# Attention and two MLPs: norm weight folded into a matrix, row-tiled transposes, one threshold on GpSimd, one addition on ScalarE

## What is computed

```python
scores = q @ k.T / 8
keep   = scores >= max(scores) - tau
attn   = where(keep, exp(scores - max), 0);  attn /= sum(attn) + 1e-9
x      = attn @ v                                     # 2304 x 512

h    = x @ w_in1                                      # 512 -> 1024
solu = h * softmax(h)
ln   = (solu - mean(solu)) / sqrt(var(solu) + 1e-6) * g_ln
y    = ln @ w_out1                                    # 1024 -> 512

m = y @ w_in2                                         # 512 -> 2048
g = max(m, 0) + log(1 + exp(-|m|))
out = g @ w_out2                                      # 2048 -> 512
```

## Time and profile before

| | us |
|---|---|
| median of 3 runs | 910.83 (910.66 to 911.72) |
| the profiled execution | 911.15 |
| its span, first to last instruction | 909.4 |
| TensorE busy | 869.7 (96%) |
| VectorE busy | 762.1 (84%) |
| ScalarE busy | 501.7 (55%) |
| GpSimd busy | 433.4 (48%) |
| mean granted TensorE clock, share of full speed | 0.994 |

### The profile page before, as it was taken

How to read it: one execution, slowest core, us unless ns; L and a number is a source line. 1 busy time by engine, 2 the same in 40 slices (tenths; PEclk the granted TensorE clock), 3 DMA queues, 4 the chain that set the end, 5 groups by cost and what they waited for, 6 DMA issues and landing times.

```text
span 909.4 us, 16546 instructions
## 1 busy us (share of the span) xinstructions
PE 869.7 (96%) x6104; PEld 726.3 (80%) x6104; DVE 762.1 (84%) x1376; ACT 501.7 (55%) x936; POOL 433.4 (48%) x449
## 2 busy tenths in 40 slices
PE   6899999999989999999998998999999999999997
PEld 4566666666667889889898897999989999899995
DVE  6999999999929754835641999999999999999997
ACT  4777877888846442433442564545545455455543
POOL 3445444447617612313311565565555556556563
PEclk9999999999999999999999899999999999999999
DMA  6813431342100000000002610000000000000000
GB/s 163 217 32 80 102 97 37 80 105 75 48 25 23 24 1 1 1 1 1 1 12 88 197 30 0 36 1 1 35 1 1 35 1 1 35 0 0 35 0 35
DMA packets 29496, 37.65 MB, mean 41 GB/s; under 512 B 3696, under 2 KB 17520, under 8 KB 29424
## 3 DMA queue, kind: packets, MB, share of 16 engines
q1 hardware_dynamic: 29024, 36.42, 14.5%
q10 hardware_dynamic: 400, 0.30, 0.1%
HBM read 31.98 MB, written 4.72 MB: 40 GB/s over the span
## 4 chain that ended last, share of the span: by engine, by line
DVE 53%; PE 35%; issue 8%; POOL 1%; ACT 1%; DMA 0%; ACTq 0%; DVEq 0%; POOLq 0%
DVE g L850 12%; PE y_ps L1044 11%; DVE ntop L710 8%; PE s_ps L942 7%; DVE g_hi L854 7%; DVE g L840 5%; PE h_ps L911 5%; DVE g_lo L856 5%; DVE g L843 5%; PE o_ps L982 4%; PE f_ps L1101 3%; PE m_ps L1020 2%; DVE x_lo L705 2%; DVE solu L807 1%; DVE st_top L793 1%
## 5 line engine op out<-in xcount | busy, mean ns | idle before, releaser
L451 POOL TENSOR_TENSOR w_lo<-w_raw,w_hi 128x512 fp32r<-128x512 f32 x96 | 129.6, 1351 | 163.6 <-ACT w_hi L632 163.6
L412 POOL TENSOR_SCALAR kept<-kept,inv 128x576 f32<-128x576 f32 x144 | 106.1, 756 | 117.9 <-DVE inv L742 117.8
L511 ACT ACTIVATE expd<-s_ps,ntop 128x576 f32<-128x576 f32 x144 | 106.3, 741 | 51.7 <-DVE ntop L710 51.7
L1020 PE MATMUL m_ps<-y_hi,w_lo 128*128 128x384 f32 x384 | 131.4, 342 | 0.0
L648 ACT ACTIVATE l<-u 128x384 f32<-128x384 f32 x96 | 50.4, 525 | 145.8 <-POOL u L459 145.8
L1020 PE MATMUL m_ps<-y_lo,w_hi 128*128 128x384 f32 x384 | 130.3, 339 | 0.0
L1020 PE MATMUL m_ps<-y_hi,w_hi 128*128 128x384 f32 x384 | 129.2, 336 | 0.0
L459 POOL TENSOR_TENSOR u<-z,consts 128x384 f32<-128x384 f32 x96 | 108.2, 1127 | 41.8 <-ACT z L641 41.7
L850 DVE TENSOR_TENSOR g<-g,l 128x384 f32<-128x384 f32 x96 | 125.7, 1309 | 2.7
L1101 PE MATMUL f_ps<-w_hi,g_hi 128*128 128x512 f32 x288 | 115.4, 401 | 8.9 <-DVE g_lo L856 8.9
L710 DVE TENSOR_REDUCE ntop<-s_ps 128x1 f32<-128x576 f32 x144 | 107.5, 757 | 14.2 <-PE s_ps L942 6.8
(11 more groups left out here) (87 smaller groups left out, 1815.1 us busy)
## 6 DMA issues: line engine op xcount, KB each, us to landing
q_sb<-q_t SPq DMA_DIRECT2D x28, 288.0 KB, 5.1
v_sb<-v_main SPq DMA_DIRECT2D x16, 256.0 KB, 3.2
stage<-w_in SPq DMA_DIRECT2D x16, 256.0 KB, 2.7
w_raw<-w_out SPq DMA_DIRECT2D x8, 512.0 KB, 4.8
out<-o_sb SPq DMA_DIRECT2D x5, 768.0 KB, 3.5
k_sb<-k_t SPq DMA_DIRECT2D x21, 144.0 KB, 4.4
stage<-w_in SPq DMA_DIRECT2D x4, 512.0 KB, 8.9
stage<-w_out SPq DMA_DIRECT2D x4, 512.0 KB, 3.7
```

The costliest lines, as they stand in the source:

```text
L412: nc.gpsimd.tensor_scalar(kept[:, tile % RING, :], kept[:, tile % RING, :], inv[:, group % 2, k:k + 1], 1.0, ALU.mult, ALU.mult).then_inc( ...
L451: nc.gpsimd.tensor_tensor(w4[1][:, n % 2, :], w4_raw[:, n % F2, :], f32(w4[0][:, n % 2, :]), ALU.subtract).then_inc(w4lo_made, 1)
L511: nc.scalar.activation(expd[:, tile % 2, :].rearrange("p (a b) -> p a b", a=2), s_ps[tile % 2][:, :, 0:HALF], ACT.Exp, bias=ntop[:, tile % ...
L1020: last = nc.tensor.matmul(m_ps[n % 4][:, 0:GC], w[:, k, (n % F2) * P:(n % F2 + 1) * P], y[odd][:, k, :], start=(k == 0 and m == 0), stop=( ...
```

## The change

Four edits are made together.

- The weight g_ln is multiplied into the rows of w_out1 (`w2_scale`, on ScalarE, in place in the stage buffers, in the last doubles of attention) before that matrix is split. VectorE's z is gone; GpSimd makes ln = (solu + nmean) * rstd in one operation. `solu` now waits for `ln_made`, and ln for `lt_made`. The gain is loaded as 128x8 near the start instead of as 128x1024 after attention.
- The transposes of the first MLP are 16 instructions on 64-row tiles, one tile's outputs in one bank of `lt_ps` and the other's in the other; `ln_hi` and `ln_lo` are addressed to match.
- In attention the second threshold of a double is made by GpSimd, with a semaphore of its own (`thresh_b`), and the reduction of the sums of even groups stands at the end of the double. The key scalings and w1's halves move on GpSimd and ScalarE.
- 1 + z of the second MLP is a ScalarE activation (Identity with bias 1) instead of a GpSimd addition.

```diff
-            for group in range(GROUPS):
+            def make_threshold_b(u):
+                pool.wait_ge(top_made, 2 * u + 2)
+                col = slice((2 * u + 1) % 4, (2 * u + 1) % 4 + 1)
+                nc.gpsimd.tensor_scalar(thresh[:, col], ntop[:, col], -1.0, tau_sb[:, 0:1], ALU.mult, ALU.subtract
+                                        ).then_inc(thresh_b, 1)
+            for u in range(DOUBLES + 1):
+                if u < DOUBLES:
+                    make_threshold_b(u)
+                for group in complete(u - 1):
+                    probabilities(group)
+                unit, step = divmod(u, PT)
+                if step == PT - 2 and unit + 1 < UNITS:
+                    scale_keys(2 * unit + 2)
+                    scale_keys(2 * unit + 3)
+                if u in W1_LOW:
+                    for m in range(2):
+                        w1_low(2 * W1_LOW.index(u) + m)
...
-                pool.wait_ge(z_made, tile + 1)
-                nc.gpsimd.tensor_tensor(ln[:, slot, :], ln[:, slot, :],
-                                        st["rstd"][:, col].broadcast_to([P, DFF1]), ALU.mult).then_inc(ln_made, 1)
+                pool.wait_ge(mean_made, tile + 1)
+                wait(pool, lt_made, tile - 1)
+                nc.gpsimd.tensor_scalar(ln[:, slot, :], solu[:, slot, :], st["nmean"][:, col], st["rstd"][:, col],
+                                        ALU.add, ALU.mult).then_inc(ln_made, 1)
...
+            def w2_scale(n):
+                src, hi, lo = staged(n)
+                act.wait_ge(stage_in[n % STAGES], 16 * (n // STAGES + 1))
+                act.wait_ge(gain_in, 16)
+                for a in range(2):
+                    m = 2 * (n - C) + a
+                    nc.scalar.activation(src[:, a, :], src[:, a, :], ACT.Copy, scale=gain[:, m:m + 1]
+                                         ).then_inc(w2_scaled, 1)
...
-                if 54 <= v < 54 + 2 * C:
-                    w1_high(v - 54)
+                if 24 <= v < 24 + 3 * C and v % 3 < 2:
+                    w1_high(2 * (v // 3 - 8) + v % 3)
+                if DOUBLES <= v < DOUBLES + F1 // 2:
+                    w2_scale(C + v - DOUBLES)
...
+            def one_plus(j, n):
+                slot = n % 2
+                act.wait_ge(z2_made, j + 1)
+                wait(act, l2_made, j - 1)
+                nc.scalar.activation(u2[:, slot, :], z2[:, slot, :], ACT.Identity, bias=consts[:, 3:4]
+                                     ).then_inc(u2_made, 1)
...
-                dve.wait_ge(thresh_made, tile + 1)
+                dve.wait_ge((thresh_a, thresh_b)[tile % 2], tile // 2 + 1)
...
+                    wait(dve, ln_made, tile - 1)
                     nc.vector.scalar_tensor_tensor(out=solu[:, slot, :], in0=h_ps[slot][:, :],
...
-                    nc.vector.scalar_tensor_tensor(out=ln[:, slot, :], in0=solu[:, slot, :],
-                                                   scalar=st["nmean"][:, col], in1=gain[:, :],
-                                                   op0=ALU.add, op1=ALU.mult).then_inc(z_made, 1)
...
                 for k in range(F1):
-                    last = nc.tensor.transpose(lt_bank(tile)[:, k * P:(k + 1) * P], ln[:, slot, k * P:(k + 1) * P],
-                                               ident[:, :])
+                    for q in range(2):
+                        last = nc.tensor.matmul(lt_bank(tile)[:, q * BANK + k * DH:q * BANK + (k + 1) * DH],
+                                                ln[halves[q], slot, k * P:(k + 1) * P],
+                                                ident[halves[q], q * DH:(q + 1) * DH], is_transpose=True,
+                                                start=(k == 0), stop=(k == F1 - 1))
```

More of the change, by code:

```diff
@@ L48 @@
 LAG_V = 6
+W1_LOW = (28, 31, 37, 40)
 BANK = 512
@@ L102, in build @@
         consts = sb("consts", [P, 5])
+        gain = sb("gain", [P, F1])
         xt = sb("xt", [P, 2 * PG * C * GC])
@@ L142, in build @@
         ln = sb("ln", [P, 2, DFF1], where=phase)
-        gain = sb("gain", [P, DFF1], where=phase)
         e1 = sb("e1", [P, 2, DFF1], where=phase)
@@ L241, in x_group, with complete @@
             return (b * PG + g) * (C * GC)
+        def complete(u):
+            return [group for group in range(GROUPS) if (GROUP * group + GROUP - 1) // 2 == u]
         def place(tile):
@@ L266, in lt_bank, with lt_halves, in_halves @@
             return h_ps[1] if isinstance(tile, int) and tile == MT - 2 else lt_ps
+        def lt_halves(tile):
+            return lt_bank(tile)[:, :].rearrange("p (q a b) -> p q a b", q=2, a=F1)
+        def in_halves(rows, k):
+            return rows[:, :, k * P:(k + 1) * P].rearrange("p a (q b) -> p q a b", q=2)
         W_ITEMS = C + F1 // 2 + F2
@@ L337, in _ @@
                 sp.dma_start(staged(n)[0], staged_source(n)).then_inc(stage_in[n], 16)
+            sp.dma_start(gain[:, :], gain_d.rearrange("(k p) -> p k", p=P),
+                         allow_slow_non_contiguous=True).then_inc(gain_in, 16)
             for unit in range(2, UNITS):
@@ L405, in _, with probabilities @@
                                             ALU.mult, ALU.mult).then_inc(k_scaled, 1)
-            for group in range(GROUPS):
+            def make_threshold_b(u):
[3 more added lines that the diff above has]
+                                        ).then_inc(thresh_b, 1)
+            def probabilities(group):
@@ L409, in _ @@
                 pool.wait_ge(inv_made, group + 1)
-                for k in range(GROUP):
-                    tile = GROUP * group + k
+                for tile in range(GROUP * group, GROUP * group + GROUP):
                     nc.gpsimd.tensor_scalar(kept[:, tile % RING, :], kept[:, tile % RING, :],
-                                            inv[:, group % 2, k:k + 1], 1.0, ALU.mult, ALU.mult
+                                            inv[:, group % 2, tile % GROUP:tile % GROUP + 1], 1.0, ALU.mult, ALU.mult
@@ L681, in _ @@
             soft(last + n, n)
-            exponential(last + n + 1, n + 1)
+            soft(last + n + 1, n + 1)
             w4_high(last + n, n)
-            logarithm(last + n + 1, n + 1)
             w4_high(last + n + 1, n + 1)
@@ L745, in _ @@
                 a, b = 2 * u, 2 * u + 1
-                done = [group for group in range(GROUPS) if (GROUP * group + 2) // 2 == u - 1]
-                if a < TILES:
+                if u < DOUBLES:
                     maximum(a)
-                for group in done:
-                    raise_sums(group)
-                if a < TILES:
+                for group in complete(u - 1):
+                    if group % 2 == 1:
+                        raise_sums(group)
+                if u < DOUBLES:
                     maximum(b)
-                    make_threshold(a)
-                    make_threshold(b)
-                for group in done:
+                    make_threshold_a(u)
+                for group in complete(u - 1):
                     invert(group)
-                if a < TILES:
+                if u < DOUBLES:
                     keep(a)
                     keep(b)
+                for group in complete(u):
+                    if group % 2 == 0:
+                        raise_sums(group)
                 if u in (68, 69):
@@ L815, in mlp1 @@
                     transposed_low(i, n - 2)
-                if within(tile, MT):
-                    dve.wait_ge(mean_made, tile + 1)
-                    wait(dve, lt_made, tile - 1)
-                    if isinstance(tile, int) and tile == 0:
-                        dve.wait_ge(gain_in, 16)
-                    nc.vector.scalar_tensor_tensor(out=ln[:, slot, :], in0=solu[:, slot, :],
-                                                   scalar=st["nmean"][:, col], in1=gain[:, :],
-                                                   op0=ALU.add, op1=ALU.mult).then_inc(z_made, 1)
                 if isinstance(i, int) and tile == MT - 1:
```

61 lines of the change are left out of this document (23 added, 38 removed).

## The result

The changed kernel takes **900.14 us** in the median of six runs (898.82 to 900.37), the kernel before beside it 910.21 (907.11 to 911.72). The ratio is 0.9887, 95% interval 0.9872 to 0.9902: 10 us faster, where 18 were forecast, and 0.14 us past the upper end of the range. A second set of five runs gave 899.46 us and 0.9886 (0.9866 to 0.9905).

The account below looks back on a forecast made before the run. TensorE was taken to bound both MLPs, VectorE's 3.39 us double attention, TensorE close second. Terms 6.2 + 0.9 + 3.5 - 0.3 + 1.0 + 2.4 + 1.7 + 2.6 = 18.0 us gave 892.8 us, range 885.5 to 900.0.

Parts of the forecast that it names:

- the threshold term: Attention: second threshold to GpSimd saves VectorE 0.13 us in two doubles of three, 6.2 us (bounds 0 and 9.2).
- Rival 4: Attention: GpSimd's threshold comes late and the second kept waits in each double; slower, 934 us at 1.3 us each; chance 0.04.
- Rival 2: Attention: ScalarE's exponential or the value products bind at once, so the threshold gains nothing; 899.0 us; chance 0.14.
- Rival 3: Second MLP: the gaps stay, VectorE's two-input operations still held up by GpSimd's w_lo; 900.5 us; chance 0.10.
- Rival 5: Whole kernel: pieces do not add up, one stage's gain is waited for in the next; near 910 us; chance 0.03.
- 1 + z on ScalarE: Second MLP gaps: 1.0 us at the first, 2.4 plus 1.7 of low clock at the second, 2.6 at the end.
- Norm weight: First MLP: shorter TensorE waits for ln_lo, 3.5 us (bounds 0 and 4.6), less 0.3 for ScalarE's scalings in attention's tail.
- Transposes: First MLP: transposes on row tiles save 0.05 us in each of 18, 0.9 us (bounds 0 and 7.1).
- The step of the second MLP: Second MLP: the steady step of 21 products stays at 4.20 us, as TensorE has no gap to give back.
- The signs: Trace observations listed beforehand as showing the forecast right (such as kept to kept of 3.26 us) or wrong.

Follow-up runs that it names:

- e4: e1 with each exponential on 384 of 576 columns from the fifth tile on; 894.23 us, one run.
- e3: Thresholds made in the first double alone, all later tiles cut with those (140 of 144 left out); 887.97 us, one run.
- e5: The changed kernel with both thresholds of a double on GpSimd from the third double on, the first two doubles' on VectorE; 888.90 us.
- e7: e1 with 1 + z back on GpSimd; 902.83 us.
- e8: e1 with the norm's weight (operation z) on VectorE again, GpSimd's two-input product and the 128x1024 load with it; 899.30 us.
- e1: The changed kernel with the second thresholds of the first two doubles on VectorE; 894.31 us.
- e2: The changed kernel with all second thresholds back on VectorE, the other three edits kept; 896.15 us.
- e6: e1 with the first MLP's transposes undone to eight of 128 rows; 894.97 us.
- e11: The kernel of e1 measured once more, on the same chip as e10; 895.81 us.
- e12: From the third double on, first threshold on GpSimd and second on VectorE (the change mirrored), first two doubles' both on VectorE; 894.63 us.
- e9: e2 with a third 128x1 operation per double on VectorE from the third double on, its result unread; 902.40 us.
- e10: The changed kernel measured once more, on the same chip as e11; 899.46 us.

## Where the prediction was wrong and where it was right, point by point

- **The step that failed is the threshold term, +6.2 us; it measured -3 to -4.** Two errors lie in it. First, the price: 0.13 us was read off the records as the length that goes (0.34 for two, 0.209 for one). The distance that counted was from the first threshold's start to `kept`, 0.30 us, and that belongs to the result of the first. The second stood within it, but for 0.04 us where an inverse follows. The rows for that were there: in the earlier trace rows `kept` begins 0.30 us after the thresholds do. What was not there is how long it would be with one alone, so the bound of 0 was right, and the value should have been taken nearer to it. In the loop 1.4 to 1.8 us came. (47 x 0.13 is 6.1, not 6.2.)
- **Second, the queue that the threshold was moved to.** The prediction names the three scalings behind it on GpSimd and leaves out the four ahead of it at the start, which wait for DMAs until 12.70 us. It priced the steady double only. Rival 4 had the mechanism (a second `kept` that waits for GpSimd), in every double and not in the first: about 4 us instead of 23 or more. In the loop GpSimd's threshold lasts 0.29 us, as even as the 0.75 of its neighbours, and nothing waits for it.
- **Rival 2** gave 899.0 us, near what came, for a reason that wasn't the one: e4 shows that the exponential does not bind at 1.67 us, and value products bind only in the third doubles. At 1.57 (e3, e5) `kept` starts 0.04 us after the exponential's end. With that hand-over taken off, the 0.17 us of the earlier trace rows were a slack of 0.13, just what e5 then used. **Rival 3**, 900.5 us, is nearer still, and its mechanism is not what happened either: the gaps did shrink. Rival 5 is out as well, since the pieces add up.
- **1 + z on ScalarE: 7.7 forecast, 8.5 measured** (7.4 in the traces). By gap: 0.9 for 1.0; the second gap all of its 2.4, less a new one of 0.46 before it; 1.8 for 2.6. The last is 0.8 smaller than meant, because TensorE then waits 0.74 us for `w_lo`, the next that is late. The rest is mostly clock. The forecast's 1.7 us tied a fall to the second gap, as the kernel before had it; in e7's trace TensorE waits 2.36 us there too and the clock stays at 1.00 from 545 to 560 us, but it is 0.91 from 880 to 900. Behind the first gap it falls for 3.4 us or not at all in the kernels that have the edit, where before it fell for 6.3; the prediction had let it fall as before.
- **Norm weight: 3.2 net forecast, 5.0 measured** (4 to 5, with the 1.5 us between two measurements). The waits for `ln_lo` fell from 4.6 to 0.7 us, those around the first three tiles too; the prediction had left these in place. Against e8 they fell from 5.3: with the shorter transposes TensorE asks sooner, as that run's rival said. The ScalarE scalings cost 0.2 us for the 0.3 forecast.
- **Transposes: 0.9 forecast, 0.7 measured** by the medians, 1.1 by the traces. The rule of the Trainium skill (TensorEngine Tiling (Array Packing), Theoretical Speedup), up to 2x, would have been 7.1 us. It didn't come, and the 0.33 us of getting into the tiled form agrees with the other rule (Key Properties there), that a change of form drains the array.
- **The step of the second MLP** stayed (4.18 us against 4.20) with VectorE at 72 of 100 us, as argued from TensorE's full stretch.
- **The signs.** Of those for right, the step of the second MLP and the full clock behind 520 us came. A `kept` to `kept` of 3.26 us did not. One wait for `ln_lo` of 0.7 us was left near the end of the first MLP, and the last gap is 0.74, not under 0.5. Of those for wrong, a second `kept` that idles for GpSimd came once, and with it a low clock at 14.6 us.

With the threshold term at -4.0 the sum would be 892.8 + 10.2 = 903.0; the other terms brought 14.2 instead of 11.8, and that is 900.6. That the time came so near to the range is luck in part: a term with the wrong sign was offset by 2.4 us that the others brought beyond their forecast, some of it clock.

## What to carry to other kernels

A small operation is worth the distance that it adds between the starts of the two instructions around it, not its record: ask whose result the next one waits for, and if it isn't this one's, moving it gains little (here 0.04 us where it was the one too many, and nothing elsewhere). If a threshold like this is to leave an engine, move the one on the dependent chain, and both ends of that chain (e5: 7.3 us of doubles where the change had 1.5). When work is put on another engine's queue, walk that queue from its first instruction and not only in the steady loop: one wait for a DMA ahead of it cost more than 69 doubles gained.

## What the runs showed of the hardware

VectorE starts 128x1 operations that don't need one another every 0.12 to 0.13 us, though each record lasts 0.20; `kept`, which needs the threshold's result through a semaphore, starts 0.30 us after it (e4), with nothing or an inverse between them. The Trainium skill (Perfetto Trace Analysis, DVE / Act Engine Instruction) says why a record is neither number: it ends when the write is acknowledged, and the semaphore's way and the next instruction's prefetch lie outside it. The trace agrees: 0.20 of record, 0.10 more to the start of the dependent one. GpSimd makes the same threshold in 0.29 to 0.31 us.

After 3.58 us without work at the start TensorE's clock was 0.50 for 3.4 us. After about 2.7 us without work ahead of the first product down of the second MLP it fell for 3.4 us in seven profiled executions (e1, e2, e5, e6, e8, e11, e12) and not in five (the changed kernel, e3, e4, e9, e10). What decides between these is open. Part of what a full clock gives there may be waited for again: in the seven, TensorE then has no wait over 0.2 us before the last gap; in four of the five it has one of 0.45 or 0.46 us, 35 to 43 us after the first, and in the fifth (e10) one of 1.06.
